# Attention values applied as column-tiled weights, probabilities normalised on GpSimd before their transpose, scores computed two pairs further ahead

## The reference

```python
# q, k, v: batch 2, heads 8, positions 768, head size 64
scores = scale * np.matmul(q, k.transpose(0, 1, 3, 2))
keep = is_global | is_local            # 8 first keys, and the 96 last ones
scores = scores + bias[None, :, :, :]  # minus slope of the head times distance
scores = np.where(keep, scores, -1000000000.0)
scores = scores - np.max(scores, axis=-1, keepdims=True)
a = np.exp(scores)
a = a / (np.sum(a, axis=-1, keepdims=True) + 1e-09)
return np.matmul(a, v).astype(np.float32)
...
x = np.ascontiguousarray(attn_out.transpose(0, 2, 1, 3)).reshape(B, S, H * D)
x = _moe_ref(x=x, **moe_kwargs)        # x @ w_in, relu, conv, gate, @ w_out
return _moe2_ref(x=x, **moe2_kwargs)
```

## Time and profile before

| what | value |
|---|---|
| median of 3 runs | 397.18 us (396.61 to 397.22) |
| the profiled execution: its own time | 396.15 us |
| its span | 394.4 us |
| TensorE busy | 384.8 us, 98% of the span |
| VectorE, ScalarE, GpSimd busy | 54%, 43%, 8% |
| bytes moved | 27.68 MB, 70 GB/s over the span |
| TensorE's granted clock | 0.999 of full speed |

### The profile page before, as it was taken

How to read it: one execution, slowest core, us unless ns; L and a number is a source line. 1 busy time by engine, 2 the same in 40 slices (tenths; PEclk the granted TensorE clock), 3 DMA queues, 4 the chain that set the end, 5 groups by cost and what they waited for, 6 DMA issues and landing times.

```text
span 394.4 us, 6076 instructions
## 1 busy us (share of the span) xinstructions
PE 384.8 (98%) x2318; PEld 350.7 (89%) x2318; DVE 214.4 (54%) x564; ACT 170.1 (43%) x358; POOL 33.5 (8%) x51
## 2 busy tenths in 40 slices
PE   7999999999999999999999999999999999999995
PEld 2778898989898889999998899999899999998884
DVE  6455365767676666977896768021584344552000
ACT  3576354545455453985516565021465211112211
POOL 2990000000000000000002121000230000000000
PEclk9999999999999999999999999999999999999999
DMA  7943232222332200333110000001034000001222
GB/s 249 360 156 116 100 89 74 75 74 88 102 94 90 61 2 2 106 109 106 54 55 0 2 0 2 0 0 36 6 109 160 1 2 0 2 0 57 80 106 85
DMA packets 11747, 27.68 MB, mean 70 GB/s; under 512 B 1473, under 2 KB 3521, under 8 KB 11713
## 3 DMA queue, kind: packets, MB, share of 16 engines
q1 hardware_dynamic: 11568, 27.23, 20.6%
q10 hardware_dynamic: 144, 0.00, 0.0%
HBM read 24.08 MB, written 3.15 MB: 69 GB/s over the span
## 4 chain that ended last, share of the span: by engine, by line
PE 91%; DVE 4%; issue 1%; ACT 1%; DMA 1%; DVEq 0%; ACTq 0%
PE bank L1387 18%; PE bank L1389 18%; PE bank L1388 18%; PE bank L1357 17%; PE bank L1329 8%; PE bank L1294 6%; PE bank L1310 4%; DVE p_sb L915 2%; PE bank L1338 2%; DMA counts<-in_n_keys 1%; DVE c_sb L950 1%; ACT p_sb L590 1%; DVE x_sb L928 1%; ACT pt_sb L597 0%; DVE denom L925 0%
## 5 line engine op out<-in xcount | busy, mean ns | idle before, releaser
L1357 PE MATMUL bank<-xT,w_hi 128*128 128x384 f32 x256 | 76.4, 358 | 0.0
L590 ACT ACTIVATE p_sb<-p_sb,row_min 128x256 f32<-128x256 f32 (+1 forms) x96 | 41.7, 485 | 41.3 <-DVE row_min L915 41.3
L915 DVE CUSTOM_DVE_ANT_0 p_sb<-bank,bias 128x256 f32<-128x256 f32 (+1 forms) x96 | 33.0, 399 | 36.1 <-PE bank L1294 33.0
L1329 PEld LDWEIGHTS bank<-v_sb,pt_sb 128*128 128x128 f32 x352 | 44.9, 191 | 4.5 <-DVE x_sb L928 3.4
L1329 PE MATMUL bank<-v_sb,pt_sb 128*128 128x65 f32 x352 | 45.6, 271 | 1.7 <-DVE x_sb L928 1.4
L1357 PEld LDWEIGHTS bank<-xT,w_hi 128*128 128x128 f32 x256 | 45.2, 189 | 2.0 <-issue 2.0
L1357 PE MATMUL bank<-xT,w_lo 128*128 128x384 f32 x128 | 45.6, 356 | 0.0
L1387 PE MATMUL bank<-g_hi,w_hi 128*128 128x386 f32 (+1 forms) x128 | 43.3, 338 | 0.0
L1389 PE MATMUL bank<-g_hi,w_lo 128*128 128x386 f32 (+1 forms) x128 | 43.2, 337 | 0.0
L1388 PE MATMUL bank<-g_lo,w_hi 128*128 128x386 f32 (+1 forms) x128 | 43.1, 337 | 0.0
L950 DVE SCALAR_TENSOR_TENSOR c_sb<-h_sb,conv_sb,c_sb 128x382 f32<-128x382 f32 (+1 forms) x64 | 39.6, 619 | 2.3
(11 more groups left out here) (93 smaller groups left out, 727.3 us busy)
## 6 DMA issues: line engine op xcount, KB each, us to landing
stage<-in_weights SPq DMA_DIRECT2D x19, 512.0 KB, 3.3
v_sb<-in_v SPq DMA_DIRECT2D x8, 390.0 KB, 3.2
k_sb<-in_k SPq DMA_DIRECT2D x8, 384.0 KB, 4.2
out_dram<-out_sb SPq DMA_DIRECT2D x12, 256.0 KB, 2.0
q_sb<-in_q SPq DMA_DIRECT2D x13, 192.0 KB, 3.1
v_sb<-in_v SPq DMA_DIRECT2D x5, 260.0 KB, 2.7
k_sb<-in_k SPq DMA_DIRECT2D x5, 256.0 KB, 3.9
v_sb<-in_v SPq DMA_DIRECT2D x1, 780.0 KB, 8.5
```

The source lines that it names most:

```text
L590: nc.scalar.activation(p_sb[:, u % SLOTS, h, 0:n], p_sb[:, u % SLOTS, h, 0:n], ACT.Exp, bias=row_min[:, u % SLOTS, h:h + 1], scale=-1.0).t ...
L915: nc.vector.tensor_tensor_reduce(out=p_sb[:, u % SLOTS, h, 0:n], in0=score_bank(u, h)[:, u % 2 * 2 * P:u % 2 * 2 * P + n], in1=bias[:, 2 * ...
L1329: last = nc.tensor.matmul(o_ps[:, 2 * tt + h, :], pt_sb[:, u % 2, h, n * P:(n + 1) * P], rows[:, h * DV:(h + 1) * DV], start=n == 0, stop= ...
L1357: last = nc.tensor.matmul(banks[5 + j % 3][:, 0:C], w, x, start=r == 0, stop=r == F1_GROUP - 1)
```

## The change

1. `weigh` exchanges the operands. v is the weights (128 rows by 64 columns, one head in each column half of the array), and 128 columns of transposed probabilities move. The result comes out with features on partitions, as `xT` needs it, so `turn_x` is gone and `normalise` as well. Two PSUM banks alternate by triples.
2. The sum of the probabilities now comes from the exponential's accumulator output. `invert_sums` on VectorE adds 1e-9 and inverts two numbers a unit; `scale_probs` on GpSimd multiplies the unit's probabilities in place, one instruction a head; `turn_probs` waits for that.
3. The scores stand two pairs of units further ahead of their transposes: at even step u those of u+4 and u+5. `SLOTS` grows from 4 to 6.
4. On GpSimd the splitting of the chunks is cut into 16 pieces of 256 columns, one in each iteration of a loop from unit 6 on, behind `scale_probs`. The tables stand in iterations 0 to 2.
5. `copy_pt` of odd units below 14 moves to VectorE (`take_pt`).
6. On SyncE one `load_pair` stands behind each of the chunks 2 to 5, where all four chunks stood ahead of those pairs.

```diff
-SLOTS = 4
+SLOTS = 6
+PIECE = 256
+PIECES = WCH // PIECE
+PIECE_FIRST = 6
...
             for n in range(2, NW1 + 2):
                 load_chunk(n)
-            for pg in range(HP + 2, ALL_TRIPLES):
+                load_pair(HP + n)
+            for pg in range(HP + NW1 + 2, ALL_TRIPLES):
                 load_pair(pg)
...
+            def scale_probs(u):
+                n = keys(u)
+                pool.wait_ge(inverted, u + 1)
+                for h in range(2):
+                    probs_h = p_sb[:, u % SLOTS, h, 0:n]
+                    nc.gpsimd.tensor_scalar(probs_h, probs_h, denom[:, u % SLOTS, h:h + 1], 1.0, ALU.mult, ALU.mult
+                                            ).then_inc(scaled, 1)
+            def split_piece(i):
+                n, part = divmod(i, PIECES)
+                cols = slice(part * PIECE, (part + 1) * PIECE)
...
+            scale_probs(0)
+            pool.wait_ge(tables, TABLE_STEPS)
+            for u in range(ALL_UNITS):
+                if u >= 1:
+                    scale_probs(u)
+                if u < HP - 1:
+                    table(2 * u + TABLE_HEADS)
+                    table(2 * u + TABLE_HEADS + 1)
+                if PIECE_FIRST <= u < PIECE_FIRST + NW1 * PIECES:
+                    split_piece(u - PIECE_FIRST)
...
-                                         bias=row_min[:, u % SLOTS, h:h + 1], scale=-1.0).then_inc(probs, 1)
+                                         bias=row_min[:, u % SLOTS, h:h + 1], scale=-1.0,
+                                         accum_out=denom[:, u % SLOTS, h:h + 1]).then_inc(probs, 1)
...
+            def invert_sums(u):
+                sums = denom[:, u % SLOTS, :]
+                dve.wait_ge(probs, 2 * u + 2)
+                nc.vector.tensor_scalar(sums, sums, 1e-9, None, ALU.add).then_inc(summed, 1)
+                dve.wait_ge(summed, u + 1)
+                nc.vector.reciprocal(sums, sums).then_inc(inverted, 1)
...
-                    pe.wait_ge(probs, 2 * u + h + 1)
+                    pe.wait_ge(scaled, 2 * u + h + 1)
...
-                for h in range(2):
-                    for n, rows in enumerate(values):
-                        last = nc.tensor.matmul(o_ps[:, 2 * tt + h, :], pt_sb[:, u % 2, h, n * P:(n + 1) * P],
-                                                rows[:, h * DV:(h + 1) * DV],
+                for n, rows in enumerate(values):
+                    for h in range(2):
+                        last = nc.tensor.matmul(xt_ps(pg)[h * D:(h + 1) * D, tt * P:(tt + 1) * P],
+                                                rows[:, h * DV:h * DV + D], pt_sb[:, u % 2, h, n * P:(n + 1) * P],
                                                 start=n == 0, stop=n == len(values) - 1)
...
-                        if u % 2 == 0 and u + 2 < ALL_UNITS:
-                            scores(u + 2)
-                        if u >= 4 and (u - 4) % TG == 0:
-                            turn_x((u - 4) // TG)
+                        if u % 2 == 0 and u + 4 < ALL_UNITS:
+                            scores(u + 4)
```

More of the change, by code:

```diff
@@ L663, in _ @@
             nc.scalar.activation(spare[:], minus_half[:], ACT.Exp, bias=minus_half[:], scale=-1.0)
-            soften(0)
+            for u in range(3):
+                soften(u)
             for u in range(STEPS):
-                if u + 1 < ALL_UNITS:
-                    soften(u + 1)
-                if u < ALL_UNITS:
+                if u < ALL_UNITS and not turned_on_dve(u):
                     copy_pt(u)
+                if u + 3 < ALL_UNITS:
+                    soften(u + 3)
                 for j in range(F1_GROUPS - KF):
@@ L1365, in _ @@
             scores(0)
+            scores(2)
             f1_next = 0
```

105 lines of the change are left out of this document (54 added, 51 removed).

## The result

| | median us | runs | profiled execution (span) |
|---|---|---|---|
| before | 397.2 | 396.61 to 397.34 | 396.15 (394.4) |
| changed | 402.94 | 401.27 to 405.0 | 403.13 (401.3) |

The ratio is 1.0147, with a 95% interval of 1.0113 to 1.018: the change made the kernel slower by 5.7 us. The forecast was 398.4 us, slower by 1.2. The side was right, the range held the time, and the size was short by 4.5 us. The four runs of the changed kernel lie 3.7 us apart, and the granted clock goes with them: 0.991 in the one of 401.27 us, 0.981 in the one of 405.0.

The account below looks back on a forecast made before the run. The prediction took TensorE's stream, busy 118.0 of 118.4 us from step 14 on, as the bound. Its terms, -4.0 - 0.4 - 2.9 + 0.5 + 8.0 = +1.2 us on 397.18, gave 398.4 us, range 390 to 405.

Parts of the forecast that it names:

- turn_x, its wait, weigh: TensorE from step 14 on: 4.0 us gained without turn_x, 0.4 without its wait, 2.9 from weigh in column halves.
- The halves take turns: In weigh, the column halves run one after the other: 11.3 us lost instead of 2.9 gained, 410.6 us; chance 0.07.
- the weight loads are not hidden in column mode: In weigh, three more exposed loads of 0.05 us in a full unit: 5.0 us lost, 403.4 us; chance 0.07.
- The stalls on loads: TensorE waits for k at odd triples 7 to 15: five stalls 6.0 us, chunks 1.0 twice, 8.0 lost.
- The front: Before step 14, where f1 joins attention: GpSimd's queue puts its start at 38.3 us, 0.5 lost, bounds 1.5 gained, 4 lost.
- The clock: Behind the five stalls, granted clock drops to 1.2 GHz: 6.9 us lost, 405.3 us; chance 0.07.
- GpSimd sets the pace: Slower GpSimd instructions and blocking: 4 us lost in front instead of 0.5, 1 to 2 later, 403.5 us; chance 0.10.
- The loads are in time: At the odd triples, k lands without stalling TensorE: 390.4 us; chance 0.29, together with cheaper switches.
- The prediction's remark that no row bears on this: On shared ports as an exclusive lock: GpSimd and VectorE never ran heavy work together in the kernel before; no size.

Follow-up runs that it names:

- e2: The kernel before with the changed weigh alone, turn_x and normalise removed, so nothing is normalised: 385.09 us, ratio 0.9709.
- e11: The changed kernel with w1 chunks 3, 4 and 5 started behind q and k of triples 7, 8 and 9 instead of ahead: 402.02 us, ratio 1.0143.
- e12: e10 with VectorE biasing one unit's scores in each step instead of two in each even step: 386.49 us, ratio 0.9733.
- e7: e1 without GpSimd's scaling of the probabilities, so not normalised: 388.4 us, ratio 0.9758.
- e1: The changed kernel with q and k started behind q and k of the triple ahead, no longer behind its v: 391.58 us, ratio 0.9864.
- e9: The changed kernel with ten matmuls of zeros ahead of the wait for k at each of five odd triples: 400.88 us, ratio 1.0099.
- e3: e1 with GpSimd's w1 pieces spread otherwise, four in units 10 to 13, two in each of 14 to 19: 392.53 us, ratio 0.99.
- e4: The changed kernel with weigh's two loops exchanged, all passes of one head before the other's: 402.58 us, ratio 1.0136.
- e5: e1 with 14 matmuls of zeros between scores(0) and scores(2), where TensorE stands: 393.06 us, ratio 0.9873.
- e6: e5 with GpSimd's pieces spread otherwise and VectorE's path tests four steps later: 389.99 us, ratio 0.9792.
- e10: e1 with the pieces and path tests of e6, and GpSimd's tables spread over units 0 to 4: 387.95 us, ratio 0.9776.

## Why the prediction was right on the side and short on the size

The terms against what was measured:

- **turn_x, its wait, weigh: -7.3.** In the stretch e2 shows -8.2. `weigh` is 0.80 us, with its halves in pairs and its loads hidden, as in the forecast. It isn't halved, because some 0.37 us of entry and exit stand beside 0.43 of streaming. *The halves take turns* and *the weight loads are not hidden in column mode* are both out; with them the rule of the Trainium skill, "TensorE: Matmul & The Clock Gate", Part 3, that a load overlaps only when its row group differs. The trace doesn't agree with it here: all column halves share one row group, and the passes of one half follow each other in 0.109 us with a load of 0.137 recorded for each. The same part of that page also has loads go ahead into a background weight buffer, which would fit; no run here tells.
- **The stalls on loads: +8.0.** Measured 7.7, at the five triples that the forecast named. The parts inside were off: the chunks were worth 1.0 us of waiting and not 2.0 (e11), and a stall without one lay between 0.7 us (triple 9 in e11) and 2.0 (triple 7 there), with 1.0 to 1.6 at the other three in the changed kernel, where I had 1.2 for each.
- **The front: +0.5, with a bound of 4.** Measured +4.2 (37.77 to 42.00). This is the step that failed, and by more than it shows: part 1 alone brings step 14 to 34.2 us (e2), so the rest of the change costs 7.8 us there. It counted GpSimd's queue in busy time from the first table on and took the other engines as covered. GpSimd's units did take 2.1 us, as forecast. But three orders were not followed through: `scores(2)` ahead of the first transpose waits for the rest of k (1.9 us at once); GpSimd has two tables in front of the scalings of units 1 and 2; and `take_pt` is queued on VectorE behind two units of bias and the path tests. With the path tests moved already, e12 takes the bias out of the way and gains 2.3 us, and e7 shows 1.6 us for the scaling. By order alone step 14 comes back to 36.9 us (e12). The front can't be split exactly, since the low clock falls in another place in nearly every one of these runs.
- **The clock: 0 in the sum, a rival with 0.07.** Measured 3.4 us behind step 14 in the profiled run; e1's `f1` stretch is 9.8 us shorter where the stalls alone are 7.7, although it has a low stretch of its own that costs 1.5, and e9 gains 1.9 with the stalls still there. It came beside the forecast's case and not in its place: a consequence of the stalls belongs into their price.
- **What wasn't in the sum:** the pair of scores that moves out of the stretch, -1.3.

Together: 1.2 + (4.2 - 0.5) + 3.4 - (8.2 - 7.3) - 1.3 - (8.0 - 7.7) = 5.8 us, against 5.7 measured. And from the other end: e2's 385.1, plus stalls 7.7, clock 3.4 and step 14's 42.0 - 34.2 = 7.8, less 1.3, is 402.7 us, against 402.9. The runs of the changed kernel alone spread over 3.7 us, so that the sums meet this closely is chance.

The side was in part luck. Without what the front and the clock took beyond the forecast, the first of these sums gives 1.2 - 0.9 - 1.3 - 0.3 = -1.3 us, a faster kernel: the gains were larger than forecast, and two losses that were counted too low outweighed them.

*GpSimd sets the pace* was wrong in its second half. VectorE's taps took longer beside it, 666 ns on average against 619 before and 619 again in e7, which leaves the scaling out. GpSimd's scaling took 372 ns (128 columns) to 775 with a median of 478, where the forecast had 400 to 520 for 256 columns. But no wait of TensorE behind step 14 comes from either. The Trainium skill, "SBUF — State Buffer", the section on two separate sides, calls the shared ports an exclusive lock; the trace shows 8% more on VectorE's taps, and single scalings of up to 775 ns, which neither prove nor exclude one. The prediction's remark that no row bears on this was wrong: between 10 and 30 us of the kernel before, GpSimd was busy for 17.8 us and VectorE for 10.4. *The loads are in time* came true only in e1, at 391.6 us, where the forecast had 390.4.

## What to carry to other kernels

When a reader is moved forward, move its load too: ask of each load which wait stands ahead of it in its queue, and whether that wait belongs to it. Here q and k waited behind a v that waited for `weigh`, and their order alone was worth 2.8%. When something is issued ahead of the first use, follow its own wait as well, at the start of the program above all, and look at what each in-order queue puts between a result and the copy that the bounding engine wants next. A stall of the bounding engine has to be priced with the clock that may fall behind it.

## What was not expected of the hardware

- **The granted clock falls behind short waits.** It was at the 1.2 GHz level behind stalls of 2.2 and 1.5 us (changed kernel, the rows from 54 and 115.5 us), and behind the wait of 1.8 to 1.9 us for VectorE's copy at 41 to 43 us (e1, e3, e4, e5, e9, e11). It stayed at 1.00 behind the same 1.9 us in the changed kernel, behind stalls of 1.5 and 1.6 us (76 and 138 us), and behind 1.1 us (e6, e10). Matmuls of zeros in a gap kept it up there, and it fell in the next row instead, at 15 to 20 us (e5).
- **The column halves don't need to alternate in the listing** (e4): 0.59 us from `weigh` to the next product in both orders.
- **The exponential's accumulator output is an instruction of its own** on ScalarE, 0.19 us for each of the 96.
